# Delta-rule attention beside a mixture of experts: the nine products of an early group in one piece instead of three

## What is computed

```python
for t in range(S):
    kt, vt, bt = (k_n[:, :, t], v[:, :, t], beta[:, :, t, None])
    y[:, :, t] = np.einsum('bhd,bhde->bhe', q[:, :, t], state)
    v_old = np.einsum('bhde,bhd->bhe', state, kt)
    state = state + bt[:, :, :, None] * np.einsum('bhd,bhe->bhde', kt, vt - v_old)
```

## Time and profile before

| | |
|---|---|
| median of three runs | 2574.24 us (2572.38 to 2574.74) |
| profiled execution, its own time | 2572.69 us |
| its span | 2570.9 us |
| mean granted clock of TensorE | 0.99 |
| busy: TensorE, VectorE, ScalarE, GpSimd | 2466.6, 1013.1, 663.9, 841.4 us |
| early products (L181), all 1152 matmuls | 282.4 us busy |
| attention's rounds with early groups | about 170 to 638 us of the span |

### The profile page before, as it was taken

The page is one execution under the profiler, slowest core; times in us unless marked ns, Lnnn a source line. Parts: engine busy times, 40 slices in busy tenths (PEclk is TensorE's granted clock), DMA queues, the critical chain, the costliest instruction groups (busy, mean ns, idle before and its releaser), DMA issues.

```text
span 2570.9 us, 42139 instructions
## 1 busy us (share of the span) xinstructions
PE 2466.6 (96%) x17923; PEld 2362.1 (92%) x17923; DVE 1013.1 (39%) x2181; ACT 663.9 (26%) x1454; POOL 841.4 (33%) x753
## 2 busy tenths in 40 slices
PE   5889999999849999999999999999999999999999
PEld 4778888888749999999999999999999999999999
DVE  5776666663513333333333333333333333333332
ACT  3344444443311111111111111111111122222222
POOL 5545555552060232033113302321331131443432
PEclk9999999999979999999999999999999999999999
DMA  2113323332220111011001101110110010000001
GB/s 78 45 63 102 107 95 108 102 105 75 68 98 2 49 50 32 18 49 50 25 25 50 50 16 35 50 42 8 50 50 25 25 50 1 25 13 13 13 19 56
DMA packets 96378, 124.58 MB, mean 48 GB/s; under 512 B 5184, under 2 KB 82240, under 8 KB 96192
## 3 DMA queue, kind: packets, MB, share of 16 engines
q1 hardware_dynamic: 96192, 121.90, 14.3%
HBM read 91.99 MB, written 29.88 MB: 47 GB/s over the span
## 4 chain that ended last, share of the span: by engine, by line
PE 73%; issue 1%; DMA 1%; POOL 0%; DVE 0%; ACT 0%; SPq 0%; ACTq 0%; DVEq 0%; POOLq 0%
PE bank L1218 39%; PE bank L1189 32%; PE bank L181 1%; PE bank L1121 1%; DMA w_raw<-in_moe_w 0%; PE bank L1167 0%; POOL w_hl L1043 0%; POOL w_hl L1037 0%; DMA h_early<-h_out 0%; DVE h_raw L1327 0%; DVE x_rest L1333 0%; ACT x_rest L1247 0%; PE bank L1107 0%; PE bank L1225 0%; ACT h_out L191 0%
## 5 line engine op out<-in xcount | busy, mean ns | idle before, releaser
L1218 PE MATMUL bank<-w_hl,h_hl 128*128 128x384 f32 x5760 | 1021.5, 334 | 34.1 <-issue 34.1
L1218 PEld LDWEIGHTS bank<-w_hl,h_hl 128*128 128x128 f32 x5760 | 1001.9, 188 | 34.4 <-issue 34.4
L1189 PE MATMUL bank<-x_rest,w_hl 128*128 128x384 f32 x4320 | 783.3, 338 | 0.0
L1189 PEld LDWEIGHTS bank<-x_rest,w_hl 128*128 128x128 f32 x4320 | 763.9, 187 | 0.0
L1371 DVE SCALAR_TENSOR_TENSOR x_tok<-bank,route,x_tok 128x384 f32<-128x384 f32 x384 | 237.2, 618 | 555.5 <-PE bank L1218 555.5
L1072 POOL TENSOR_TENSOR h_hl<-h_raw,h_hl 128x384 fp32r<-128x384 f32 x128 | 125.9, 1016 | 947.8 <-ACT h_hl L1268 947.8
L1276 ACT ACTIVATE h_hl<-bank 128x384 fp32r<-128x384 f32 x384 | 189.0, 492 | 946.0 <-PE bank L1189 946.0
L1349 DVE SCALAR_TENSOR_TENSOR h_hl<-bank,h_hl 128x384 fp32r<-128x384 f32 x384 | 214.2, 558 | 437.6 <-ACT h_hl L1276 437.6
L181 PE MATMUL bank<-x_first,w_hl 128*128 128x384 f32 x1152 | 282.4, 363 | 0.7 <-ACT h_out L191 0.7
L1093 POOL TENSOR_TENSOR h_hl<-h_raw,h_hl 128x384 fp32r<-128x384 f32 x128 | 129.6, 1017 | 296.5 <-ACT h_hl L1286 296.5
L181 PEld LDWEIGHTS bank<-x_first,w_hl 128*128 128x128 f32 x1152 | 188.5, 191 | 11.4 <-issue 10.3
(11 more groups left out here) (116 smaller groups left out, 1813.6 us busy)
## 6 DMA issues: line engine op xcount, KB each, us to landing
w_raw<-in_moe_w SPq DMA_DIRECT2D x48, 768.0 KB, 4.9
h_early<-h_out SPq DMA_DIRECT2D x128, 192.0 KB, 1.9
h_raw<-h_early SPq DMA_DIRECT2D x32, 768.0 KB, 6.1
kq_t<-in_kq_rows SPq DMA_DIRECT2D x48, 256.0 KB, 3.0
kv<-in_kv_cols SPq DMA_DIRECT2D x24, 384.0 KB, 3.9
out<-x_tok SPq DMA_DIRECT2D x8, 576.0 KB, 3.0
w_raw<-in_moe_w_in SPq DMA_DIRECT2D x4, 768.0 KB, 4.6
w_raw<-in_moe_w_out SPq DMA_DIRECT2D x4, 768.0 KB, 4.5
```

The source lines that it names most:

```text
L1189: m = pe.matmul(bank[:, f, 0:TB], w1_hl[hn % 2][:, a, kc, f * P:(f + 1) * P], x_at(c, kc, b * TB, TB), start=n + kc == 0, stop=n == len(PA ...
L1218: m = pe.matmul(bank[:, 4 + t, 0:DM], h_hl[:, b % 2, a, f, t * P:(t + 1) * P], w2_hl[hn % 2][:, c, f, :], start=n + f == 0, stop=n == len( ...
```

## The change

`early` loses its argument `part`. A group's nine matmuls are issued in one call, at six places of the round instead of thirds at 18. The turns of tokens use the same function, so they move with it. The order on ScalarE, VectorE, GpSimd and SyncE, the slots, the banks and the table stay as they are.

```diff
-                        def early(k, part):
+                        def early(k):
 
                             at = G * NPAIR + i
                             if (item := early_slot(at, k)) is None:
                                 return
-                            if part == 0 and (last := slot_before(at, k)) is not None:
+                            if (last := slot_before(at, k)) is not None:
...
-                            if item[0] == "up":
+                            if item[0] == "turn":
+                                turn_early(item[1], BE + k % 2)
+                                return
+                            for part in range(KC):
                                 early_part(pe, item[1], part, BE + k % 2)
-                            elif part == 0:
-                                turn_early(item[1], BE + k % 2)
...
                         chain(0, key_state)
                         levels(1, level_y)
-                        early(0, 0)
                         prep(0, grams)
-                        early(0, 1)
+                        early(0)
                         levels(1, level_x)
                         levels(1, level_xt)
-                        early(0, 2)
                         chain(0, solve, True)
-                        early(1, 0)
                         levels(2, level_y)
-                        early(1, 1)
+                        early(1)
                         chain(0, product)
-                        early(1, 2)
                         levels(2, level_x)
                         levels(2, level_xt)
-                        early(2, 0)
                         chain(0, correct)
-                        early(2, 1)
+                        early(2)
                         levels(3, level_y)
-                        early(2, 2)
                         prep(0, first_x)
-                        early(3, 0)
                         chain(0, outputs, True)
                         levels(3, level_x)
-                        early(3, 1)
+                        early(3)
                         chain(1, key_state)
                         levels(3, level_xt)
-                        early(3, 2)
                         levels(4, level_y)
-                        early(4, 0)
                         prep(1, grams)
-                        early(4, 1)
+                        early(4)
                         levels(4, level_x)
                         levels(4, level_xt)
-                        early(4, 2)
                         chain(1, solve, True)
                         levels(5, level_y)
-                        early(5, 0)
                         chain(1, product)
-                        early(5, 1)
+                        early(5)
                         levels(5, level_x)
                         levels(5, level_xt)
-                        early(5, 2)
                         chain(1, correct)
```

## The result

The changed kernel takes 2642.88 us (median of four runs, 2640.67 to 2645.12) against 2574.49 before (2572.38 to 2576.87, four runs): ratio 1.0265, interval 1.0248 to 1.0283. The direction was as forecast, the size was not: +68.4 us where the sum said +49.6, and 0.9 us beyond the upper end of the range.

What follows compares the result with a forecast made beforehand. TensorE, over 90% busy, was taken as the bound, with thirds covering its hand-overs. About +2.8 us a round over 15 full rounds (42), plus first, last and token-turning rounds, gave +49.6: 2622 us, range 2602 to 2642.

Steps and rivals of the forecast that it cites:

- the thirds are the cover: Thirds of groups fill TensorE's hand-overs to copying engines; moving them loses about 3.9 us a round in uncovered hand-overs.
- seven stretches: Parts of one round between fixed TensorE points, each priced separately; together +2.7 to +2.8 us a round.
- Stretch 6: Fourth xt to end of second product: 0 change, since TensorE waits there for ScalarE's chain anyway; between -0.3 and +0.3.
- the price of an entry: Coming to a group from another kind of product costs TensorE 0.09 us; 12 fewer entries save 1.1 us a round.
- The rival that only this would remain: Waits only take up slack, leaving the saved entries: 18 us less, 2554 us; chance 0.03.
- the reorder window: TensorE's queue pulls weight loads ahead; if it hid every load, entries would be free and the sum 1.1 us a round worse.
- I cost it at nothing: Half clock after the new TensorE waits of 0.3 to 1.2 us, priced at zero because similar rounds keep 1.00.
- The half-speed rival: The clock falls in every round, 2.4 us each over 17 rounds: 41 us on top, 2663 us; chance 0.06.
- stretch 3: Product to outputs: 5.12 us become 4.5, -0.6, with correct starting 2.15 us behind the product's start.
- 0.4 later: One end for the residual of product to outputs, where VectorE is late; the other end was 0.2 earlier.
- the last rounds: Attention's end: the 15th full round +2.8 us, the last but one +2.8, the last, with the chain alone, +0.6.
- Time behind 640 us: Sign of being wrong: extra time behind 640 us, as everything behind the attention should stay as long as before.

Runs made afterwards that it cites:

- e2: The changed kernel with the fourth group of a round back in thirds at its three old places: 2632.75 us, ratio 1.0235.
- e3: The changed kernel with groups 1 to 5, still nine matmuls in one piece, each placed in a hand-over on TensorE: 2565.74 us, ratio 0.9966.
- e4: e3 plus ScalarE copying z0 ahead of the Relu and weight cast beside it, in both halves of a round: 2544.67 us, ratio 0.989.
- e5: The changed kernel with only ScalarE's z0 copy moved ahead of the Relu and weight cast, TensorE's order untouched: 2617.00 us, ratio 1.0166.
- e7: e4 with two of a round's six groups split, one third ahead of solve and two behind it: 2547.74 us, ratio 0.9903.
- e1: The changed kernel with 14 dummy matmuls ahead of each round's second product, from round 6 on: 2628.81 us, ratio 1.0216.
- e8: The changed kernel with 14 dummy matmuls ahead of each round's first correct instead of the second product, from round 6 on: 2646.37 us, ratio 1.0279.
- e9: e1 with GpSimd holding the squares, and all behind them, until VectorE has written the first chunk's residual: 2628.07 us, ratio 1.0209.

## Why the prediction was right, and where it was wrong

**Right: the thirds are the cover.** The lengths of the uncovered hand-overs were taken from rounds without early groups, and six of seven stretches came out within 0.05 us. e2 gave 10 us back with one group's thirds, and e3 and e4 show that nine in one piece are no disadvantage by themselves: inside the hand-overs they beat the thirds. So it was their place, as argued. Stretch 6 was right too: with ScalarE's chain untouched nothing changes there (3.25 us both times), and with z0 first (e5) it does.

**Right: the price of an entry**, 0.09 us by the rows, 0.10 by e7. The rival that only this would remain, and the kernel become faster, fell as the waits showed. What the prediction says of the reorder window stands in the table at the head of the Trainium skill's page "TensorE: Matmul & The Clock Gate" and not in the section that it names; e7 agrees with its reading that an entry is not free.

**Wrong: "I cost it at nothing", said of a clock of half speed.** This is the term that carried the result out of the range. In 7 of 14 rounds the sixth group ran at half clock, 10.1 us in all. I had looked at each wait by itself (0.3 to 1.2 us) and at rounds without early groups that hold the clock. But the rounds of the earlier trace rows have dummy matmuls exactly ahead of the product, and my reading of them named the dummies and drew nothing from them. In the changed kernel openings stand close together there: 0.36 and 0.20 us ahead of the fifth y, and 0.83 or 0.32 ahead of the product, with little between them. e1 shows that filling the last is enough, e5 that closing it is, and e8 that filling another is not. Why seven rounds fell and the seven others, with the same waits, did not is open. The half-speed rival had priced a fall in every round, 41 us, and was given 0.06; the truth was a fall in half of them, at 1.4 us each. The Trainium skill, "TensorE: Matmul & The Clock Gate", section "Why this matters for your kernels", does warn of idle gaps between matmuls, but of gaps longer than any wait of these rounds; the prediction stretched that rule when it read the new waits into it. The trace agrees that idle time takes the clock, and goes further: waits of 0.83 us and less were followed by half clock.

**Mis-sized: stretch 3.** 4.71 us instead of 4.5. `correct` started 2.37 us behind the product instead of the 2.15 that I took. The residual needed 0.28 us more because VectorE's last instruction ran beside GpSimd's squares (e9). In the rounds from which I took 2.15 us other work of GpSimd stood there. The text had kept "0.4 later" as an end. The rounds without a fall came to 3.06 instead of 2.8, over 14 of them 3.6 us more.

**Mis-sized: the last rounds.** From the 15th full round to the end +9.4 instead of 6.2. The 15th took 3.7 more instead of 2.8, because its first `correct` waits longer than the 0.91 us of the others; VectorE's last instruction takes 1.08 us there:

```profile
638.66 0.37 PE L464 MATMUL bank<-res_hl,xx 128*128 128x48 bf16 x8 [1.35 <-DVE res_hl L742]
```

The last but one took 2.9 more, as priced (2.8). The last took 1.2 instead of 0.6: it has no levels between the products, so that the second product, which I had priced as nearly covered, waits 1.09 us, and the first `correct` starts 2.09 us behind its product with no other work between. The remaining 1.5 us came behind the attention, where the clock fell once more, for 3.4 us at 706.4 us; e1, without that fall, has +7.6 from the 15th round on. Time behind 640 us was a sign of being wrong that the prediction had named.

**Not shown to be the change's: the start.** 3.3 us of the profiled execution's difference came from matmuls that ran slow for longer in one early round. It adds up: 49.6 forecast, 10.1 clock in the 14 rounds, 3.6 rounds, 1.7 waits at the end, 1.5 clock behind the attention, 3.3 start, and -0.5 in round 6 and the turned tokens, 69.3.

## What to carry to other kernels

Where an in-order engine hands work to another and back, measure the bare length of the hand-over, and place independent work of just that length inside it; how finely the work is cut matters less than where it stands. Before a wait is costed by its length alone, look what idle time stands near it: short openings in a row took TensorE's clock here, and cheap matmuls that nobody reads paid for themselves. A small copy on which the in-order engine waits belongs ahead of the bulk work on the copying engine.

## What was not expected of the hardware

14 dummy matmuls of 128 x 128 in one gap of 1.1 us kept the clock at 1.00 through 14 rounds at 88% busy, while the same dummies in a gap elsewhere left it at 0.93 to 0.97 at 89% busy. A single wait of 1.06 us behind a full group and one `level_y` took no clock in e3, and three of 0.36, 0.20 and 0.83 us within 2 us of each other did in half of the rounds. A VectorE instruction of 0.36 us took 0.64 us beside a GpSimd instruction on f32 data, and 0.36 again when that one was held back. In round 6 one wait of 2.4 us was followed by 5 us at 0.52 of the clock, while two waits of 0.76 and 0.89 us in the same place, with 0.9 us of products between them, were not.
